# Late value products of key chunks 0 and 1 as three one-pass products of high and low halves, in an attention and mixture-of-experts kernel on one core

## The chip, the cores and the metric

One core of a Trainium2 chip. The metric is the device time of one execution in microseconds (us). Engines are named as the profile names them: PE is TensorE (PEld its weight loads), DVE VectorE, ACT ScalarE, POOL GpSimd, SP the queue that issues DMAs.

## The reference

32 heads (4 batches of 8) of 576 positions and 64 dimensions go through attention with a mask of 64-wide blocks; the result goes through a gated MLP with a one-step token shift, and then through a mixture of 8 experts of which each token uses one.

```python
    scores = scale * np.matmul(q, k.transpose(0, 1, 3, 2))
    mask = block_i >= block_j            # blocks of 64 positions
    scores = np.where(mask, scores, -1000000000.0)
    attn = np.exp(scores - np.max(scores, axis=-1, keepdims=True))
    attn = attn / (np.sum(attn, axis=-1, keepdims=True) + 1e-09)
    x = np.matmul(attn, v)               # then 512 wide per token
...
    k = np.maximum(xk @ w_k, 0.0)        # xk, xr: x mixed with the token before
    x = (1.0 / (1.0 + np.exp(-(xr @ w_r)))) * (k * k @ w_v)
...
    h = np.maximum(x[b, s] @ w1[e], 0.0)
    out[b, s] = p[e] * (h @ w2[e])
```

## The kernel before, in words

The program has three stages one behind the other: attention (32 heads, the first 200 us or so), the MLP, the experts. Each engine has its own hand-written order of instructions, and semaphores alone tie them together; nothing is scheduled by a planner. The change is in the attention stage.

A head `i` has five key chunks: four of 128 keys and one of 64. Its queries are 576 columns. Scores are made transposed (keys on partitions, queries along the row), so that chunk `c` needs only queries from `128 c` on. In PE's order, head `i` runs:

- `head_scores(i, ...)` (L708, L709): per piece one product of the rounded halves `hi` and one of `aug` (the low half of q, the row maximum and the mask), both in the one-pass type fp32r. The five pieces are chunk 0 for queries 0 to 255, chunk 0 from 256 on, chunk 1 (448 columns), chunk 2 (320 columns), and chunks 3 and 4 (192 and 64 columns).
- between them `head_row(i + 1)` (L694), which turns the row maxima of head i+1 into a row, and `head_max(i + 2, ...)` (L683, L686): rough scores of head i+2 in four groups, from which DVE takes the row maxima. Group 3 (L686, two products of 288 columns) goes into banks that groups 0 and 1 used, so it waits until DVE has reduced group 1.
- `head_pv(i, ...)` (L730): the product of the values with the exponentials, in full fp32. `PV` lists its seven products as (chunk, from query, to query); the early ones (queries under 256) and the late ones (from 256 on) go to two PSUM banks.

ACT in head `i`: `copy_out(i-1, 1)` (L1080) takes the late bank of the head before to `o_raw`; `head_exp(i)` (L1059) makes `pT`, the exponentials, in five pieces; `cast_tops(i+3)` (L1095) rounds q and k of head i+3 into `aug`; `split_wm_hi` (L1089) rounds a piece of an MLP weight (heads 4 to 30); `copy_out(i, 0)` takes the early bank. DVE: `copy_row(i+1)` (L1284), reductions (L1273, L1276) of the rough scores of head i+2 out of PSUM, `split_wm_lo` (L1308, heads 5 on), `cast_hi(i+3)` (L1295) and `split_q_lo(i+3)` (L1300), which read SBUF, a reciprocal of the sums (L1289). POOL: `split_k(i+3)` (L517), low half of k, after DVE's L1300 of that head; then `normalise(i-3)` (L526), which multiplies the output of head i-3 with its inverse sums into `xT`. SP issues the loads; the inverse sums go through DRAM (`spread_sums`, `store_inv`, `load_inv`).

`head_pv` waits for `row_copied` of head i+1, and `head_row(i+1)` for the maxima of that head, so a late DVE holds PE at those places and at group 3 of `head_max`.

Of the kernel before, what the change touches and what calls it, by code (L numbers as in the profile page):

```python
# [5 lines left out]
F32 = mybir.dt.float32  # L6
# [3 lines left out]
R32 = mybir.dt.float32r  # L10
ALU = mybir.AluOpType
ACT = mybir.ActivationFunctionType
AX = mybir.AxisListType
P = 128


def attention_moe_program(nc, qkT, v, mu_k, mu_r, w_k, w_v, w_r, w_gate9, w1, w2, out):

    NHEAD, _, _, S = qkT.shape
    DH = qkT.shape[1] // 2  # L20
# [7 lines left out]
    CH = (S + P - 1) // P  # L28
# [25 lines left out]
    with ExitStack() as ctx:  # L54
# [53 lines left out]
        mark = top["work"]  # L108
# [3 lines left out]
        P_AT = [sum(S - P * j for j in range(c)) for c in range(CH + 1)]  # L112
# [6 lines left out]
        v_sb = place("work", "v_sb", [P, 2, CH, 4 * DH])  # L119
# [5 lines left out]
        sums = place("work", "sums", [BLK, 2, S // BLK])  # L125
        inv = place("work", "inv", [P, S])
        pT = place("work", "pT", [P, 2, P_AT[CH]])
        attention_end, top["work"] = top["work"], mark

        xm = [[None, None], [None, None]]  # L130
        xm[0][1] = place("work", "xm_k_lo", [P, DC, NT], R32)
# [13 lines left out]
        assert max(top["work"], attention_end) <= top["w_mlp"] - 4 * DC * NT  # L145
        top["work"] = top["w_mlp"] - 4 * DC * NT
        xm[0][0] = place("work", "xm_k_hi", [P, DC, NT], R32)
        top["work"] = mark

        top["x"] = x_mark  # L150
# [124 lines left out]
        def third_at(j):  # L275
# [3 lines left out]
        ps = psum("ps", [P, 8, 512])  # L279


        names = ("pool_set const_done aug_made aug_copied aug_masked aug_set tops_cast hi_cast q_split k_split max_scores max_reduced max_row row_copied "
                 "scores_t exp_done pv_done o_copied sums_chain norm_done wm_is_hi wm_split xm_tmp xm_summed xm_is_hi "
                 "xm_split k_done relu_done ksq_done ksq_is_hi ksq_split r_done rexp_done sig_done v_done y_done "
                 "rows_done lg_sums logits_read ytok_done chain pre_dve pre_pe first_known slot_0 slot_1 ranks_read rt_dve rt_pe rt_exp shifted p_known p_stored slots_known exps_known turns_known tables o_half "
                 "weights_ready we_is_hi we_split xgt_ps xgt_is_hi xgt_done h_done relu_h ht_ps ht_is_hi ht_done "
                 "o_done o_scaled idx_copied waits_alone mu_loaded xm0_is_hi xm0_split").split()
        (pool_set, const_done, aug_made, aug_copied, aug_masked, aug_set, tops_cast, hi_cast, q_split, k_split, max_scores, max_reduced, max_row, row_copied,
         scores_t, exp_done, pv_done, o_copied, sums_chain, norm_done, wm_is_hi, wm_split, xm_tmp, xm_summed,
         xm_is_hi, xm_split, k_done, relu_done, ksq_done, ksq_is_hi, ksq_split, r_done, rexp_done, sig_done, v_done, y_done,  # L290
         rows_done, lg_sums, logits_read, ytok_done, chain, pre_dve, pre_pe, first_known, slot_0, slot_1, ranks_read, rt_dve, rt_pe, rt_exp, shifted, p_known, p_stored, slots_known, exps_known, turns_known,
         tables, o_half, weights_ready, we_is_hi, we_split, xgt_ps, xgt_is_hi, xgt_done, h_done, relu_h, ht_ps, ht_is_hi,
# [3 lines left out]
        def two(name):  # L296
            return [sem(f"{name}{k}") for k in range(2)]

        qk_loaded, v_loaded, row_loaded, sums_spread, inv_stored, inv_loaded = [
            two(n) for n in ("qk_loaded", "v_loaded", "row_loaded", "sums_spread", "inv_stored", "inv_loaded")]  # L300
# [49 lines left out]
        MAXB, OUTB = 3, 6  # L350
# [150 lines left out]
        def _(pool):  # L501
# [2 lines left out]
            nc.gpsimd.affine_select(out=ident[:, :], in_=ident[:, :], pattern=[[-1, P]], compare_op=ALU.not_equal,  # L504
                                    fill=1.0, base=0, channel_multiplier=1).then_inc(const_done, 1)
            nc.gpsimd.memset(xT[:, :, 0:1], 0.0)
            nc.gpsimd.memset(v_sb[:, :, :, :].rearrange("p j c (a d) -> p (j c) a d", d=DH)[:, :, 0:4:3, :], 1.0).then_inc(pool_set, 1)

            def alone():
# [3 lines left out]
            def split_k(i):  # L513

                pool.wait_ge(q_split, i + 1)
                alone()
                nc.gpsimd.tensor_tensor(hi[i % NBUF][DH:P, KEY, :], qk_raw[DH:P, i % 2, 1, :],  # L517
                                        hi[i % NBUF][DH:P, KEY, :].bitcast(F32), ALU.subtract).then_inc(k_split, 1)
                pool.wait_ge(k_split, i + 1)

            def normalise(i):

# [12 lines left out]
            pool.wait_ge(pool_set, 3)  # L535

            for i in range(NHEAD):
                if i + NBUF < NHEAD:
                    split_k(i + NBUF)
                if i >= NBUF:  # L540
                    normalise(i - NBUF)
# [27 lines left out]
            for bb in range(B):  # L569
                at, grp = bb * S % G, bb * S // G  # L570
# [95 lines left out]
        def _(pe):  # L666
            mm = nc.tensor.matmul
# [47 lines left out]
            def head_pv(i, pieces):  # L715
# [4 lines left out]
                for k in pieces:  # L720
# [11 lines left out]
                    if k in (2, 6):  # L732
                        last.then_inc(pv_done, 1)

            pe.wait_ge(const_done, 2)
            pe.wait_ge(aug_set, 1)
            head_max(0, (0, 1, 2, 3))
            head_row(0)
            pe.wait_ge(aug_copied, 16 * (NBUF - 1))
            head_max(1, (0, 1, 2, 3))  # L740
            for i in range(NHEAD):
                ahead = i + 2 < NHEAD
                head_scores(i, (0, 1))
                if i + 1 < NHEAD:
                    head_row(i + 1)
                if ahead:
                    head_max(i + 2, (0,))
                head_scores(i, (2, 3, 4))
                if ahead:
                    head_max(i + 2, (1,))  # L750
                head_pv(i, (0, 1))
                if ahead:
                    head_max(i + 2, (2,))
                head_pv(i, (2, 3))
                if ahead:
                    head_max(i + 2, (3,))
                head_pv(i, (4, 5, 6))
# [299 lines left out]
        def _(act):  # L1057
# [6 lines left out]
            def head_exp(i):  # L1064

                wait(act, pv_done, 2 * (i - 1))
                for j, piece in enumerate(PIECES):
                    act.wait_ge(scores_t, 5 * i + j + 1)
                    for c, q0, q1, col in piece:
                        rows, at = min(P, S - c * P), P_AT[c] - c * P  # L1070
                        last = exp(pT[0:rows, i % 2, at + q0:at + q1], ps[0:rows, PBANK[j], col:col + q1 - q0], scale=SCALE)
                    last.then_inc(exp_done, 1)

            def copy_out(i, half):

# [186 lines left out]
        def _(dve):  # L1262
# [101 lines left out]
            def xm_lo(s, w):  # L1364
# [2 lines left out]
                vec.tensor_tensor(xm[w][1][:, :, :], xsum[w][:, :, :], xm[w][0][:, :, :].bitcast(F32),  # L1367
                                  ALU.subtract).then_inc(xm_split, 1)

            for i in range(NHEAD):  # L1370
                if i + 1 < NHEAD:
                    copy_row(i + 1)
                if i + 2 < NHEAD:
                    head_reduce(i + 2, 0)
                if WFIRST < i:
                    split_wm_lo(i - 1 - WFIRST)
                if i + NBUF < NHEAD:
                    cast_hi(i + NBUF)
# [402 lines left out]
```

## Time and profile before

| | |
|---|---|
| median of 3 runs | 785.57 us (783.55 to 785.67) |
| the profiled execution | 783.86 us |
| its span, first to last instruction | 782.1 us |
| mean granted TensorE clock | 0.992 |
| PE, PEld busy | 96%, 84% of the span |
| DVE, ACT, POOL busy | 61%, 45%, 23% of the span |

A line of the profile names the source line, engine, operation, output tile and input tiles. A matmul in fp32 is recorded as two matmuls with their own weight loads; one in fp32r as one. The starts of matmuls are measured and their ends are modelled, so the distance from one start to the next tells what a matmul costs.

### The profile page before, as it was taken

The page shows a single profiled execution, that of the slowest core. Times are in us where ns is not written, and L with a number is a line of the kernel's source. Part 1 is how long each engine was busy: PE and PEld are TensorE (multiplying, and loading weights), DVE is VectorE, ACT ScalarE, POOL GpSimd, SP SyncE. Part 2 cuts the span into 40 slices and gives each one's busy share as a digit, 9 for nine tenths or more (in the row PEclk, how much of TensorE's full clock was granted, in tenths as well). Part 3 has the DMA queues.
Part 4 walks back from the last instruction along what each step waited for, and adds up shares of the span by engine and source line. Part 5 has one row for each costly group of instructions (what it writes and reads, how often), then busy time and mean ns, then how long its engine had stood idle before and what let it go on. Part 6 is the DMA issues. An engine that isn't in the chain of part 4 may idle for free.

```text
span 782.1 us, 13312 instructions
## 1 busy us (share of the span) xinstructions
PE 752.9 (96%) x4026; PEld 656.9 (84%) x4027; DVE 476.4 (61%) x848; ACT 350.3 (45%) x673; POOL 182.5 (23%) x211
## 2 busy tenths in 40 slices
PE   5999999999999999999999999989999999999993
PEld 4788788777889999999999998778888788888882
DVE  8777777878487775848478696622223745453261
ACT  4677677766662625335161333122123644353350
POOL 3244554454200000000020000123223232323221
PEclk9999999999999999999999999999999999999997
DMA  5666756552000010010101071167110176431000
GB/s 163 202 188 183 226 191 183 176 155 72 24 9 1 1 41 1 1 40 1 41 1 41 1 263 47 41 232 280 41 32 27 40 254 231 148 135 39 27 13 9
DMA packets 43061, 74.39 MB, mean 95 GB/s; under 512 B 10061, under 2 KB 20470, under 8 KB 43012
## 3 DMA queue, kind: packets, MB, share of 16 engines
q1 hardware_dynamic: 38676, 64.30, 24.5%
q0 software_dynamic: 4336, 9.47, 3.5%
q8 instruction: 27, 0.44, 0.2%
q14 instruction: 22, 0.18, 0.1%
HBM read 65.31 MB, written 10.57 MB: 97 GB/s over the span
## 4 chain that ended last, share of the span: by engine, by line
PE 93%; DVE 3%; ACT 1%; issue 1%; ACTq 0%; POOL 0%; DVEq 0%; POOLq 0%
PE ps L777 21%; PE ps L778 21%; PE ps L779 21%; PE ps L730 12%; PE ps L708 4%; PE ps L709 3%; PE ps L683 3%; PE ps L923 2%; PE ps L767 2%; PE ps L686 2%; PE ps L844 1%; ACT we_hi L1201 1%; PE ps L694 0%; DVE negm L1273 0%; DVE ksq L1354 0%
## 5 line engine op out<-in xcount | busy, mean ns | idle before, releaser
L730 PE MATMUL ps<-pT,v_sb 128*128 128x320 f32 (+4 forms) x448 | 112.4, 374 | 0.0
L730 PEld LDWEIGHTS ps<-pT,v_sb 128*128 128x128 f32 (+1 forms) x448 | 76.6, 193 | 19.1 <-issue 8.0
L777 PE MATMUL ps<-we_hi,hT_hi 128*128 (+1 forms) x176 | 73.3, 417 | 2.0 <-DVE o_sb L1727 1.3
L777 PE MATMUL ps<-we_hi,xgT_hi 128*128 (+1 forms) x176 | 70.4, 400 | 1.4 <-issue 1.4
L778 PE MATMUL ps<-we_lo,xgT_hi 128*128 (+1 forms) x176 | 69.7, 396 | 0.0
L779 PE MATMUL ps<-we_hi,xgT_lo 128*128 (+1 forms) x176 | 69.6, 395 | 0.0
L778 PE MATMUL ps<-we_lo,hT_hi 128*128 (+1 forms) x176 | 69.4, 394 | 0.0
L779 PE MATMUL ps<-we_hi,hT_lo 128*128 (+1 forms) x176 | 69.3, 394 | 0.0
L1222 ACT ACTIVATE hT_hi<-ps 128x512 fp32r<-128x512 f32 x44 | 26.1, 598 | 94.4 <-PE ps L923 50.5
L517 POOL TENSOR_TENSOR hi<-qk_raw,hi 64x576 fp32r<-64x576 f32 x32 | 44.8, 1401 | 96.7 <-DVE aug L1300 96.5
L777 PE MATMUL ps<-xm_k_hi,wk_hi 128*128 128x384 f32 x192 | 65.2, 340 | 1.6 <-DVE ksq L1414 1.6
L777 PE MATMUL ps<-ksq_hi,wv_hi 128*128 128x384 f32 x192 | 66.0, 344 | 0.7 <-DVE yT L1449 0.7
L1059 ACT ACTIVATE pT<-ps 128x256 f32<-128x256 f32 (+2 forms) x192 | 61.0, 391 | 9.6 <-PE ps L709 9.3
L778 PE MATMUL ps<-ksq_lo,wv_hi 128*128 128x384 f32 x192 | 64.9, 338 | 0.0
L779 PE MATMUL ps<-ksq_hi,wv_lo 128*128 128x384 f32 x192 | 64.9, 338 | 0.0
L779 PE MATMUL ps<-xm_k_hi,wk_lo 128*128 128x384 f32 x192 | 64.6, 336 | 0.0
L778 PE MATMUL ps<-xm_k_lo,wk_hi 128*128 128x384 f32 x192 | 64.4, 335 | 0.0
L1620 DVE TENSOR_TENSOR we_lo<-we_raw,we_hi (+1 forms) x48 | 55.6, 1219 | 10.9 <-ACT we_hi L1201 10.9
L1435 DVE RECIPROCAL sig<-sig 128x384 f32<-128x384 f32 x24 | 61.3, 2553 | 0.8
L1159 ACT ACTIVATE relu_k<-ps 128x384 f32<-128x384 f32 x48 | 23.6, 491 | 81.0 <-PE ps L779 81.0
L708 PE MATMUL ps<-hi 128*128 128x256 f32 (+2 forms) x192 | 56.4, 311 | 1.9 <-ACT pT L1059 1.9
L1633 DVE TENSOR_TENSOR hT_lo<-ps,hT_hi 128x512 fp32r<-128x512 f32 x44 | 30.0, 685 | 44.2 <-ACT hT_hi L1222 44.2
(254 smaller groups left out, 1676.1 us busy)
## 6 DMA issues: line engine op xcount, KB each, us to landing
we_raw<-w SPq DMA_DIRECT2D x12, 2048.0 KB, 11.7
qk_raw<-qkT SPq DMA_DIRECT2D x32, 576.0 KB, 3.8
v_sb<-v SPq DMA_DIRECT2D x16, 320.0 KB, 5.1
inv<-inv_scratch SPq DMA_DIRECT2D x32, 144.0 KB, 4.4
y_scratch<-ytok SPq DMA_DIRECT2D x6, 768.0 KB, 3.4
wk_raw<-w_k SPq DMA_DIRECT2D x8, 256.0 KB, 5.3
wv_raw<-w_v SPq DMA_DIRECT2D x8, 256.0 KB, 4.9
wr_raw<-w_r SPq DMA_DIRECT2D x4, 256.0 KB, 4.9
```

The source lines that it names most:

```text
L517: nc.gpsimd.tensor_tensor(hi[i % NBUF][DH:P, KEY, :], qk_raw[DH:P, i % 2, 1, :], hi[i % NBUF][DH:P, KEY, :].bitcast(F32), ALU.subtract).th ...
L708: mm(dst, hi[b][:, KEY, keys], hi[b][:, Q, q0:q1], start=True, stop=False)
L730: last = mm(ps[:, OUTB + half, q0 - 256 * half:q1 - 256 * half], v_sb[0:rows, j % 2, c, cols], pT[0:rows, i % 2, at + q0:at + q1], start=( ...
L777: mm(dst, a_hi, b_hi, start=(k == 0), stop=False)
L778: mm(dst, a_hi, b_lo, start=False, stop=False)
L779: return mm(dst, a_lo, b_hi, start=False, stop=(k == n - 1))
L1059: return nc.scalar.activation(dst, src, ACT.Exp, **kw)
L1159: nc.scalar.activation(relu_k[:, f % 2, :], ps[:, KB + f % 2, 0:NT], ACT.Relu).then_inc(relu_done, 1)
L1222: nc.scalar.activation(hT_hi[:, half * FC // 2:(half + 1) * FC // 2, :].rearrange("p f t -> p (f t)"), ps[:, 3 + half, :], ACT.Copy).then_ ...
L1435: vec.reciprocal(sig[:, d, :], sig[:, d, :]).then_inc(sig_done, 1)
L1620: vec.tensor_tensor(we_lo[part][:, third], we_raw[part][:, third], we_hi[part][:, bass.ds(slot_at(j) + k * EPIECE, EPIECE)].bitcast(F32), ...
L1633: vec.tensor_tensor(hT_lo[:, fs, :].rearrange("p f t -> p (f t)"), ps[:, 3 + half, :], hT_hi[:, fs, :].rearrange("p f t -> p (f t)").bitca ...
```

## The change

For heads 0 to 27 (`NSPLIT`) the two late products of chunks 0 and 1 (320 queries each) are no longer one fp32 product each. The exponentials and the values are written as a high half (rounded to fp32r) and a low half (the rest), and each product becomes three fp32r products: high by high, low by high, high by low. The low by low part is left out. ACT makes the high half of the exponentials (`p_hi`), POOL the low half in place (`pT_lo` lies on `pT`), DVE both halves of the values once per pair of heads. The late bank is now begun by chunk 2, and the six new products come last in the head, behind group 3 of `head_max`. Line numbers of the changed kernel are larger: L709 and L712 there are L683 and L686 here, L734 and L735 are L708 and L709, L775 and L782 are L730.

```diff
+            def split_p(i):
+                for c in range(2):
+                    pool.wait_ge(p_is_hi, 2 * i + c + 1)
+                    alone()
+                    nc.gpsimd.tensor_tensor(late_half(pT_lo, i)[:, c, :], late_half(pT, i)[:, c, :], p_hi[:, c, :].bitcast(F32),
+                                            ALU.subtract).then_inc(p_split, 1)
+                    pool.wait_ge(p_split, 2 * i + c + 1)
...
             for i in range(NHEAD):
+                if i < NSPLIT:
+                    split_p(i)
                 if i + NBUF < NHEAD:
                     split_k(i + NBUF)
...
+            def head_pv_late(i):
+                cols, end = slice((1 - i % 2) * P, (1 - i % 2) * P + P), ps[:, OUTB + 1, 0:LATE]
+                pe.wait_ge(v_split, i // 2 + 1)
+                for c in range(2):
+                    pe.wait_ge(p_split, 2 * i + c + 1)
+                    mm(end, v_hi[:, c, cols], p_hi[:, c, :], start=False, stop=False)
+                    mm(end, v_hi[:, c, cols], late_half(pT_lo, i)[:, c, :], start=False, stop=False)
+                    last = mm(end, v_lo[:, c, cols], p_hi[:, c, :], start=False, stop=(c == 1))
+                last.then_inc(pv_done, 1)
...
+                if i < NSPLIT:
+                    head_pv_split(i, (0, 1))
+                    head_max(i + 2, (2,))
+                    head_pv_split(i, (2, 3, 4))
+                    head_max(i + 2, (3,))
+                    head_pv_late(i)
+                    continue
                 head_pv(i, (0, 1))
...
                     last.then_inc(exp_done, 1)
+                    if i < NSPLIT and j in (2, 3):
+                        act.wait_ge(exp_done, 5 * i + j)
+                        nc.scalar.activation(p_hi[:, j - 2, :], late_half(pT, i)[:, j - 2, :], ACT.Copy).then_inc(p_is_hi, 1)
...
+            def split_v(j):
+                wait(dve, pv_done, 4 * j)
+                dve.wait_ge(v_loaded[j % 2], 16 * (j // 2) + 16)
+                mine = slice(DH, 3 * DH)
+                vec.tensor_copy(v_hi[:, :, mine], v_sb[:, j % 2, 0:2, mine]).then_inc(v_is_hi, 1)
+                dve.wait_ge(v_is_hi, j + 1)
+                vec.tensor_tensor(v_lo[:, :, mine], v_sb[:, j % 2, 0:2, mine], v_hi[:, :, mine].bitcast(F32),
+                                  ALU.subtract).then_inc(v_split, 1)
             for i in range(NHEAD):
+                if i % 2 == 0 and i < NSPLIT:
+                    split_v(i // 2)
                 if i + 1 < NHEAD:
                     copy_row(i + 1)
```

The other new lines are `head_pv_split`, the same fp32 products without the two late ones (chunk 0 now in one piece for queries under 256), new buffers, four more memsets of POOL at the start (the columns of ones and zeros of `v_hi` and `v_lo`), and PE's wait for them.

The order of instructions shows the new places. PE, from the early value products to the scores of the next head, before:

```order
L730 MATMUL ps<-pT,v_sb 128x256
L730 MATMUL ps<-pT,v_sb 128x320
L683 MATMUL ps<-aug_71 128x512
L730 MATMUL ps<-pT,v_sb 128x128
L730 MATMUL ps<-pT,v_sb 128x320
L686 MATMUL ps<-aug_71 64x288 x2
L730 MATMUL ps<-pT,v_sb 128x320
L730 MATMUL ps<-pT,v_sb 128x192
L730 MATMUL ps<-pT,v_sb 128x64
L708 MATMUL ps<-hi_68 128x256
```

and of the change, from group 2 of the rough scores on:

```order
L709 MATMUL ps<-aug_71 128x512
L782 MATMUL ps<-pT,v_sb 128x320
L782 MATMUL ps<-pT,v_sb 128x192
L782 MATMUL ps<-pT,v_sb 128x64
L712 MATMUL ps<-aug_71 64x288 x2
L791 MATMUL ps<-p_hi,v_hi 128x320
L792 MATMUL ps<-pT_lo,v_hi 128x320
L793 MATMUL ps<-p_hi,v_lo 128x320
L791 MATMUL ps<-p_hi,v_hi 128x320
L792 MATMUL ps<-pT_lo,v_hi 128x320
L793 MATMUL ps<-p_hi,v_lo 128x320
L734 MATMUL ps<-hi_68 128x256
```

Two fp32 products of 320 columns are gone, six one-pass ones stand at the end, and group 3 of the rough scores has all the fp32 products before it. POOL in the steady state of the heads, before:

```order
L517 TENSOR_TENSOR hi_72<-qk_raw,hi_72 64x576
L526 TENSOR_TENSOR xT<-o_raw,inv 64x576
L517 TENSOR_TENSOR hi_68<-qk_raw,hi_68 64x576
L526 TENSOR_TENSOR xT<-o_raw,inv 64x576
L517 TENSOR_TENSOR hi_70<-qk_raw,hi_70 64x576
```

and of the change:

```order
L541 TENSOR_TENSOR pT_lo<-pT,p_hi 128x320 x2
L532 TENSOR_TENSOR hi_72<-qk_raw,hi_72 64x576
L550 TENSOR_TENSOR xT<-o_raw,inv 64x576
L541 TENSOR_TENSOR pT_lo<-pT,p_hi 128x320 x2
L532 TENSOR_TENSOR hi_68<-qk_raw,hi_68 64x576
```

Each head has two more subtractions on POOL, ahead of the two it had. DVE in an even head of the change, from its first new row:

```order
L1447 CAST v_hi<-v_sb 128x2x128
L1449 TENSOR_TENSOR v_lo<-v_sb,v_hi 128x2x128
L1356 CAST m_rows<-ps 5x128
L1345 TENSOR_REDUCE negm<-ps 128x1 x2
L1380 TENSOR_TENSOR wk_lo<-wk_raw,wk_hi 128x374
L1367 CAST hi_70<-qk_raw 128x1152
L1372 TENSOR_TENSOR aug_71<-qk_raw,hi_70 64x576
L1345 TENSOR_REDUCE negm<-ps 128x1 x2
```

The first two rows are new, ahead of the copy of the row of maxima; the rest is as before.

## Rows read from the trace of the kernel before

**Rows 1.** The chain that ended last, by engine; the stretch of heads by windows.

```profile
PE 93%; DVE 3%; ACT 1%; issue 1%; ACTq 0%; POOL 0%; DVEq 0%; POOLq 0%
12.00:170.00 158.00, 157.74 (x868) 125.83 (x869) 120.74 (x260) 110.06 (x259) 71.58 (x52) 1.00 0.59 186
```

**Rows 2.** Timeline of PE in one head: start us, us, engine, line.

```profile
151.22 0.39 PE L708 MATMUL ps<-hi 128*128 128x256 f32 x1
...
152.21 0.37 PE L708 MATMUL ps<-hi 128*128 128x448 f32 x1
152.42 0.37 PE L709 MATMUL ps<-aug 69*128 69x448 f32 x1
...
153.47 1.13 PE L730 MATMUL ps<-pT,v_sb 128*128 128x256 f32 x4
154.20 0.63 PE L683 MATMUL ps<-aug 69*128 69x512 f32 x1
154.67 0.93 PE L730 MATMUL ps<-pT,v_sb 128*128 128x128 f32 x4
155.48 0.48 PE L686 MATMUL ps<-aug 69*64 69x288 f32 x2
...
157.12 0.39 PE L708 MATMUL ps<-hi 128*128 128x256 f32 x1
```

**Rows 3.** Timeline of DVE in the same head.

```profile
152.13 0.28 DVE L1284 CAST m_rows<-ps 5x128 fp32r<-5x128 f32 x1 [1.27 <-PE ps L694]
...
152.95 0.54 DVE L1308 TENSOR_TENSOR wv_lo<-wv_raw,wv_hi 128x374 fp32r<-128x374 f32 x1
153.42 0.76 DVE L1295 CAST hi<-qk_raw 128x1152 fp32r<-128x1152 f32 x1
154.21 0.75 DVE L1300 TENSOR_TENSOR aug<-qk_raw,hi 64x576 fp32r<-64x576 f32 x1
154.89 1.14 DVE L1273 TENSOR_REDUCE negm<-ps 128x1 fp32r<-128x384 f32 x2
...
156.07 0.69 DVE L1276 TENSOR_REDUCE negm<-ps 64x1 fp32r<-64x576 f32 x1
```

**Rows 4.** Timeline of POOL in the same head.

```profile
155.13 1.40 POOL L517 TENSOR_TENSOR hi<-qk_raw,hi 64x576 fp32r<-64x576 f32 x1 [2.88 <-DVE aug L1300]
156.74 1.41 POOL L526 TENSOR_TENSOR xT<-o_raw,inv 64x576 f32<-64x576 f32 x1 [0.20 <-POOL hi L517]
```

**Rows 5.** Timeline of ACT in the same head.

```profile
151.33 0.53 ACT L1080 ACTIVATE o_raw<-ps,eps 128x320 f32<-128x320 f32 x1 [1.41 <-PE ps L730]
...
152.82 1.19 ACT L1059 ACTIVATE pT<-ps 128x448 f32<-128x448 f32 x4 [0.28 <-PE ps L709]
...
154.95 0.51 ACT L1089 ACTIVATE wv_hi<-wv_raw 128x374 fp32r<-128x374 f32 x1
155.35 0.47 ACT L1080 ACTIVATE o_raw<-ps,eps 128x256 f32<-128x256 f32 x1
```

**Rows 6.** POOL by line and shape: a narrow operation.

```profile
L534 POOL TENSOR_SCALAR omu<-mu 128x8 f32<-128x8 f32 x1 | 0.5, 506 | 1.0 <-DMA idw<-w_gate 1.0
```

**Rows 7.** Timelines of POOL and DVE where the two meet, first meeting.

```profile
187.85 1.43 POOL L526 TENSOR_TENSOR xT<-o_raw,inv 64x576 f32<-64x576 f32 x1 [0.20 <-POOL xT L526]
188.34 1.34 DVE L1308 TENSOR_TENSOR wv_lo<-wv_raw,wv_hi 128x374 fp32r<-128x374 f32 x1
```

**Rows 8.** The same, second meeting.

```profile
204.88 1.09 DVE L1361 TENSOR_TENSOR xm_k_lo<-ksq,xm_k_hi 128x384 fp32r<-128x384 f32 x2
205.48 1.76 POOL L526 TENSOR_TENSOR xT<-o_raw,inv 64x576 f32<-64x576 f32 x1 [4.34 <-DMA inv<-inv_scratch]
```

**Rows 9.** PE after a long wait, and the windows (PE, PEld, DVE, ACT, POOL, PEclk, DMA share, GB/s) behind it.

```profile
195.65 0.41 PE L708 MATMUL ps<-hi 128*128 128x320 f32 x1 [1.86 <-ACT pT L1059]
197.00:199.00 2.00, 2.00 (x7) 1.51 (x6) 1.53 (x4) 0.49 (x2) 0.00 (x0) 0.50 0.23 76
199.00:201.00 2.00, 2.00 (x9) 1.34 (x8) 0.00 (x0) 1.48 (x3) 1.25 (x1) 0.83 0.00 0
```

More of the change, by code:

```diff
@@ L127, in attention_moe_program, with late_half @@
         pT = place("work", "pT", [P, 2, P_AT[CH]])
-        attention_end, top["work"] = top["work"], mark
+        NSPLIT = NHEAD - 4
+        LATE = S - 256
+        pT_lo = nc.alloc_sbuf_tensor_at("pT_lo", [P, 2, P_AT[CH]], R32, offset=top["work"] - 4 * 2 * P_AT[CH])
+        attention_end = top["work"]
+        p_hi = place("work", "p_hi", [P, 2, LATE], R32)
+        v_hi = place("work", "v_hi", [P, 2, 4 * DH], R32)
+        v_lo = place("work", "v_lo", [P, 2, 4 * DH], R32)
+        split_end, top["work"] = top["work"], mark
+        def late_half(tile, i):
+            return tile[:, i % 2, 256:256 + 2 * (S - P)].rearrange("p (c q) -> p c q", c=2)[:, :, 0:LATE]
         xm = [[None, None], [None, None]]
@@ L147, in attention_moe_program @@
         xm[0][0] = place("work", "xm_k_hi", [P, DC, NT], R32)
+        assert split_end <= top["work"]
         top["work"] = mark
@@ L282, in attention_moe_program @@
         names = ("pool_set const_done aug_made aug_copied aug_masked aug_set tops_cast hi_cast q_split k_split max_scores max_reduced max_row row_copied "
-                 "scores_t exp_done pv_done o_copied sums_chain norm_done wm_is_hi wm_split xm_tmp xm_summed xm_is_hi "
+                 "scores_t exp_done p_is_hi p_split v_split v_is_hi pv_done o_copied sums_chain norm_done wm_is_hi wm_split xm_tmp xm_summed xm_is_hi "
                  "xm_split k_done relu_done ksq_done ksq_is_hi ksq_split r_done rexp_done sig_done v_done y_done "
@@ L288, in attention_moe_program @@
         (pool_set, const_done, aug_made, aug_copied, aug_masked, aug_set, tops_cast, hi_cast, q_split, k_split, max_scores, max_reduced, max_row, row_copied,
-         scores_t, exp_done, pv_done, o_copied, sums_chain, norm_done, wm_is_hi, wm_split, xm_tmp, xm_summed,
+         scores_t, exp_done, p_is_hi, p_split, v_split, v_is_hi, pv_done, o_copied, sums_chain, norm_done, wm_is_hi, wm_split, xm_tmp, xm_summed,
          xm_is_hi, xm_split, k_done, relu_done, ksq_done, ksq_is_hi, ksq_split, r_done, rexp_done, sig_done, v_done, y_done,
@@ L506, in _ @@
             nc.gpsimd.memset(xT[:, :, 0:1], 0.0)
+            for half in (0, 3):
+                nc.gpsimd.memset(v_hi[:, :, half * DH:half * DH + DH].bitcast(F32), 1.0)
+                nc.gpsimd.memset(v_lo[:, :, half * DH:half * DH + DH].bitcast(F32), 0.0)
             nc.gpsimd.memset(v_sb[:, :, :, :].rearrange("p j c (a d) -> p (j c) a d", d=DH)[:, :, 0:4:3, :], 1.0).then_inc(pool_set, 1)
@@ L733, in head_pv, with head_pv_split @@
                         last.then_inc(pv_done, 1)
+            def head_pv_split(i, pieces):
+                j, cols = i // 2, slice((1 - i % 2) * P, (1 - i % 2) * P + P)
+                early, end = ps[:, OUTB, :], ps[:, OUTB + 1, 0:LATE]
+                for c in pieces:
+                    if c == 0:
+                        pe.wait_ge(v_loaded[j % 2], 16 * (j // 2) + 16)
+                        pe.wait_ge(row_copied, min(i + 2, NHEAD))
+                        wait(pe, o_copied, 2 * i - 1)
+                    if c == 2:
+                        wait(pe, o_copied, 2 * i)
+                    at = P_AT[c] - c * P
+                    if c < 2:
+                        pe.wait_ge(exp_done, 5 * i + (1, 3)[c])
+                        last = mm(early[:, c * P:256], v_sb[:, j % 2, c, cols], pT[:, i % 2, at + c * P:at + 256],
+                                  start=(c == 0), stop=(c == 1))
+                        if c == 1:
+                            last.then_inc(pv_done, 1)
+                    else:
+                        rows, q0 = min(P, S - c * P), max(256, c * P)
+                        pe.wait_ge(exp_done, 5 * i + (4, 5, 5)[c - 2])
+                        mm(end[:, q0 - 256:], v_sb[0:rows, j % 2, c, cols], pT[0:rows, i % 2, at + q0:at + S],
+                           start=(c == 2), stop=False)
+            def head_pv_late(i):
[6 more added lines that the diff above has]
+                    last = mm(end, v_lo[:, c, cols], p_hi[:, c, :], start=False, stop=(c == 1))
+                last.then_inc(pv_done, 1)
             pe.wait_ge(const_done, 2)
             pe.wait_ge(aug_set, 1)
+            pe.wait_ge(pool_set, 2)
             head_max(0, (0, 1, 2, 3))
```

## The prediction

> **What bounds the kernel now.** I read the chain of waits first: 93% of it is PE, and in the stretch of heads PE is busy 157.74 of 158.00 us, DVE 120.74, ACT 110.06 and POOL 71.58 [rows 1]. So TensorE sets the attention stage, and an edit that shortens PE pays only while the others keep up. Next the timeline of PE: one head lasts from 151.22 to 157.12, that is 5.90 us [rows 2]. In the others' timelines of that head, DVE waits 1.27 us for the row product, ACT 1.41 and 0.28 us, POOL 2.88 us for L1300 [rows 3 to 5]. By time alone there is room for new work. The last view is where operations of DVE and POOL meet, because busy shares don't show what two engines do to each other [rows 7, 8].
>
> **PE's own gain.** Below I count from the head's start, 151.22. From 153.47 to 154.67 stand fp32 products of 256 and 320 columns and one of 512 in one pass; the one-pass rate is 0.21 us for 448 columns (152.21 to 152.42), 0.47 ns per column, so that 0.24 of the 1.20 us is the 512, and 0.96/576 = 1.67 ns per column is the fp32 rate. From 154.67 to 155.48 it is 0.81/448 = 1.81 [rows 2]. The two late products therefore cost 1.07 to 1.16 us, and six one-pass ones of 320 columns 6 x 0.15 = 0.90. The gain is 0.17 to 0.26 us per head; I take 0.22, which would be 28 x 0.22 = 6.2 us if nothing else moved. The weight loads stay behind products of this width; the order of the other products moves them, and I cost that at nothing (cover: the products of 288 and 320 columns in front of the new ones).
>
> **ACT.** Two copies of 320 columns: L1089, 374 columns, takes a slot of 0.40 us (154.95 to 155.35), so 0.35 each, 0.70 per head against 1.69 us of waits [rows 5]. The exponentials of chunks 3 and 4 come 0.7 us later, near 3.5, and their products stand at 3.6 or later: hidden. If that cover were gone, it would cost a few tenths of a us in every head.
>
> **POOL.** A subtraction of 576 columns takes 1.40 us [rows 4]. In proportion 320 columns are 0.78. A narrow operation of 8 columns takes 0.51 us [rows 6]; if that much were fixed, 320 columns would cost 0.51 + 0.89 x 320/576 = 1.00. I take 0.80, nearer to the rows of the same operation. POOL then works 2 x 0.80 + 1.40 + 1.41 = 4.4 us per head, by itself under 5.7. DVE gets in each even head a cast of 256 columns (0.76/1152 ns per column and some start: 0.25) and a subtraction of 256 (0.54 for 374 columns: 0.40). The four memsets and PE's new wait at the start lie in time in which POOL waits anyway: nothing. SP's queue keeps its transfers and order; its waits on POOL's split and on the inverse sums have the time of a head in hand.
>
> **What the two do to each other.** This is the step that decides. At 188.34 a subtraction of DVE with both inputs in SBUF takes 1.34 us in place of 0.54, while a multiplication of POOL runs to 189.28 [rows 7, 3]: it got going 0.14 us before POOL's recorded end (189.68 - 0.54 = 189.14). The other way round, POOL's operation at 205.48 takes 1.76 in place of 1.41, beside a DVE pair that ends at 205.97 [rows 8, 4]. They don't share; one stands until the other is done, all but some 0.13 us. In the steady head of before this never shows: POOL's two operations (3.91 to 5.31, 5.52 to 6.93) lie beside reductions from PSUM, and L1308, L1295 and L1300 are done at 3.74 [rows 3, 4]. The new POOL operations come at 2.5, when ACT has the high halves, right in the middle of L1295 and L1300.
>
> No row shows a cast (L1295, L1447) meet POOL, so its price lies between nothing and the whole. It goes through a column in 0.66 ns (0.76/1152), the subtraction next to it in 1.30 (0.75/576) [rows 3]: twice the rate, which suggests that it too uses the second way to SBUF. I take the whole. The Trainium skill, page SBUF — State Buffer, section Who interferes with whom, says that VectorE and GpSimd share one port pair as an exclusive lock, held by VectorE operations with two SBUF inputs and by fp32 copies and casts in the two-port mode; by that rule the cast counts in full, as I count it, and a reader who keeps only to the rows has the rival on the casts below.
>
> The sum of what excludes each other, per pair of heads: DVE 2 x (0.54 + 0.76 + 0.75) + 0.25 + 0.40 = 4.75; POOL 2 x (1.40 + 1.41 + 1.60) = 8.82; together 13.6, or 6.8 us per head. (Before: 2.05 + 2.81 = 4.86 of 5.90, so it fitted.) With some 0.13 us saved at each of about ten handovers the floor is 6.15. So **the shared access becomes the bound** in place of PE.
>
> By the chain, in an odd head: row copy at 0.9 and L1308 on time; the cast 2.2 to 2.9, first split 2.8 to 3.6, L1300 3.5 to 4.2, second split 4.1 to 4.9, reduction of group 1 done at 4.7, group 3 of the rough scores at 4.7 (before: 4.26), then 0.32 + 0.90: 5.95. In an even head: DVE begins with the two v operations and copies the row at 1.05 to 1.33; the normalisation left over from the head before holds the port from 1.0 to 2.3, L1308 follows to 2.8, first split 2.7 to 3.5, cast to 4.1, second split to 4.8, L1300 to 5.4, group 1 reduced at 5.87, group 3 at 5.9, end at 7.1. The mean is 6.5. Between the chain (6.5) and the plain sum (6.8) I take 6.65 for heads 5 to 27: 23 x 0.75 = 17.3. Heads 0 to 4 have no L1308; without its 0.54 the chain gives about 5.95: 5 x 0.05 = 0.3. Heads 28 to 31 are as before. Sum: +17.6 on the profiled execution, 783.86 + 17.6 = 801.5. That execution lies 1.7 us under the median of the runs, 785.57; against the median it is 803. A measurement of this kernel can tell about 0.3%, 2.4 us, from no change.
>
> **The rivals.**
> - *The forecast, the port as the bound (0.62).* Its own range: 6.15 per head (+6) to 6.8 with splits of 1.00 us (6.8 + 0.4 = 7.2, 23 x 1.3 = +30 us): 791 to 816.
> - *The casts don't hold the port, or the engines fall into an order that hides it (0.15).* Then per pair 2 x 1.29 + 0.40 + 8.82 = 11.8, 5.9 per head with nothing saved, 5.3 with the handovers; PE's path of 5.68 decides again below that. In full: -6.2, 779.4, faster; half way: no change. It decides from the point where the reduction of group 1 is done before 4.4. For it: no row shows the cast meet POOL, and DVE and POOL both have waits now. Against: even without the casts the two subtractions of DVE meet two of POOL's in a place that had none. Faster 0.10, the same 0.05.
> - *The clock falls too (0.18).* PE waited 1.86 us before 195.65, and soon after the granted clock was 0.50 (1.2 in place of 2.4 GHz) for all of 197 to 199 and 0.83 on the mean of 199 to 201 [rows 9]: 2.0 + 2.0 x 0.17/0.50 = 2.7 us at half rate, and more ahead of 197. The even head of the chain makes PE wait 5.9 - 4.4 = 1.4 us. If each of 14 such waits brings 2.7 us or somewhat more at half rate, it loses 1.4 to 1.8 us of work, up to +25 on the forecast in all, less what PE had to wait anyhow: 815 to 828. For it: the row. Against: the wait is shorter, and PE is dense around it.
> - *Late exponentials or another chain (0.05):* a wait of 0.1 to 0.2 us per head on ACT or POOL eats the gain, with the port harmless: 785 to 790, slower by a little.
>
> That the change doesn't do what it says is no rival: the order shows six one-pass products in place of two fp32 ones in each of 28 heads.
>
> **How the numbers follow.** The likeliest case gives 803. The range 788 to 824 leaves out the faster case, the same, and the upper end of the clock case, together about 2 in 10. Faster 0.10, the same 0.05, slower 0.85.
>
> **What would show it.** In the profile of the changed kernel: spacing near 0.15 us for the new products; POOL's splits recorded longer than 0.8 us, or L1295 and L1300 (now L1367 and L1372) longer than 0.76 and 0.75 or late, on a mean of two heads; PE waiting in front of group 3 of the rough scores for a DVE reduction; even heads longer than odd ones by about 1 us; a granted clock of 1.00 from 20 to 200 us, else the clock rival. I am wrong if PE stays busy without gaps there and a head lasts 5.7 us, or if PE waits in front of the new products for POOL and not in front of group 3.

## The result, and the profile after

| | before | after |
|---|---|---|
| median of 4 runs | 785.53 us (783.55 to 785.67) | 809.68 us (807.05 to 815.42) |
| the profiled execution, its span | 783.86 us, 782.1 us | 807.05 us, 805.3 us |
| mean granted clock | 0.992 | 0.986 |
| ratio | | 1.0327, 95% interval 1.0305 to 1.0349 |

The change makes the kernel 3.3% slower. The last copy of a row of maxima, which DVE makes in head 30, starts at 194.3 us before and at 217.1 after; what follows takes 587.8 and 588.1 us. So 22.8 of the 23.1 us by which the span grows lie in the heads. The tile of that copy by name, of before and of after (count, shortest, median and longest in ns, first and last start in us):

```profile
L1284 DVE CAST m_rows<-ps x32: 271/279/280, 9.5 to 194.3; 5x128 fp32r<-5x128 f32 x32
```

```profile
L1356 DVE CAST m_rows<-ps x32: 271/278/281, 9.5 to 217.1; 5x128 fp32r<-5x128 f32 x32
```

The four executions of the changed kernel are spread wider than those of before, and the two longest, 812.14 and 815.42 us, have the lowest mean granted clocks, 0.981 and 0.978; they left no trace, so more is not known of them.

Below, **us per head** is the distance from the copy of the row of head 5 to that of head 27, over 22: (169.83 - 39.93)/22 = 5.905 before, (191.14 - 41.48)/22 = 6.80 after.

The chain of work that ended last, of after (93% PE and 3% DVE in [rows 1]):

```profile
PE 76%; DVE 19%; issue 2%; ACT 1%; ACTq 0%; POOL 0%; DVEq 0%; POOLq 0%
```

A fifth of the path is now DVE. PE in after, from the end of an odd head through an even one (135.42 to 142.79) and an odd one (to 148.72): start us, us, engine, line, and in brackets the wait in front (before: [rows 2]).

```profile
134.21 0.48 PE L712 MATMUL ps<-aug 69*64 69x288 f32 x2 [0.31 <-DVE negm L1345]
134.54 0.31 PE L791 MATMUL ps<-p_hi,v_hi 128*128 128x320 f32 x1
134.68 0.31 PE L792 MATMUL ps<-pT_lo,v_hi 128*128 128x320 f32 x1
...
135.42 0.28 PE L734 MATMUL ps<-hi 128*128 128x256 f32 x1
...
141.59 0.48 PE L712 MATMUL ps<-aug 69*64 69x288 f32 x2 [1.75 <-DVE negm L1345]
...
142.79 0.28 PE L734 MATMUL ps<-hi 128*128 128x256 f32 x1
...
148.72 0.28 PE L734 MATMUL ps<-hi 128*128 128x256 f32 x1
```

The new products are 0.15 us apart as costed. PE waits in front of group 3 of the rough scores, 0.31 us in the odd head and 1.75 in the even one, for DVE's reduction of group 1. DVE and POOL beside it, DVE first (before: [rows 3, 4]):

```profile
135.62 0.57 DVE L1447 CAST v_hi<-v_sb 128x256 fp32r<-128x256 f32 x1
136.22 0.43 DVE L1449 TENSOR_TENSOR v_lo<-v_sb,v_hi 128x256 fp32r<-128x256 f32 x1
136.57 0.27 DVE L1356 CAST m_rows<-ps 5x128 fp32r<-5x128 f32 x1
...
137.30 1.09 DVE L1380 TENSOR_TENSOR wr_lo<-wr_raw,wr_hi 128x410 fp32r<-128x410 f32 x1
138.31 1.42 DVE L1367 CAST hi<-qk_raw 128x1152 fp32r<-128x1152 f32 x1
139.77 1.30 DVE L1372 TENSOR_TENSOR aug<-qk_raw,hi 64x576 fp32r<-64x576 f32 x1
```

```profile
136.24 1.71 POOL L550 TENSOR_TENSOR xT<-o_raw,inv 64x576 f32<-64x576 f32 x1 [0.20 <-POOL hi L532]
138.15 0.97 POOL L541 TENSOR_TENSOR pT_lo<-pT,p_hi 128x320 fp32r<-128x320 f32 x1 [0.20 <-POOL xT L550]
139.32 1.13 POOL L541 TENSOR_TENSOR pT_lo<-pT,p_hi 128x320 fp32r<-128x320 f32 x1 [0.20 <-POOL pT_lo L541]
141.23 1.42 POOL L532 TENSOR_TENSOR hi<-qk_raw,hi 64x576 fp32r<-64x576 f32 x1 [0.78 <-DVE aug L1372]
```

These rows show one of the two engines at work at a time, in turns. The cast L1367, 0.76 us before, takes 1.42 and ends at 139.73; less its own 0.76 it got going at 138.97, 0.15 before the recorded end of POOL's split at 139.12. L1372 takes 1.30 in place of 0.75. POOL's normalisation takes 1.71 in place of 1.41, beside `v_lo`. The same by group, of after (behind the bar the busy us and the mean ns of one; the means of L1372 and L1367 were 751 and 757 before):

```profile
L541 POOL TENSOR_TENSOR pT_lo<-pT,p_hi 128x320 fp32r<-128x320 f32 x56 | 59.8, 1067 | 31.5 <-ACT p_hi L1144 23.1 <-POOL pT_lo L541 5.7 <-POOL xT L550 2.5
L1372 DVE TENSOR_TENSOR aug<-qk_raw,hi 64x576 fp32r<-64x576 f32 x32 | 38.9, 1215 | 1.1
L1367 DVE CAST hi<-qk_raw 128x1152 fp32r<-128x1152 f32 x32 | 31.8, 993 | 1.0 <-PE ps L735 0.8
```

### The profile page after: what moved, and what is told of

It is laid out like the page before. It is cut to its first block, busy times and chain, and to the rows that moved or that the text cites. A ratio compares the mean times of both kernels' runs of the same rounds, so it can differ in the third digit from the quotient of the medians.

```text
span 805.3 us, 13666 instructions
## 1 busy us (share of the span) xinstructions
PE 750.6 (93%) x4082; PEld 666.8 (83%) x4083; DVE 518.9 (64%) x876; ACT 368.0 (46%) x729; POOL 247.4 (31%) x271
## 4 chain that ended last, share of the span: by engine, by line
PE 76%; DVE 19%; issue 2%; ACT 1%; ACTq 0%; POOL 0%; DVEq 0%; POOLq 0%
PE ps L846 20%; PE ps L848 19%; PE ps L847 19%; DVE aug L1372 5%; DVE hi L1367 4%; DVE negm L1345 3%; PE ps L992 2%; PE ps L836 2%; PE ps L712 2%; PE ps L734 1%; PE ps L735 1%; PE ps L756 1%; DVE sig L1519 1%; PE ps L913 1%; PE ps L793 1%
## 5 line engine op out<-in xcount | busy, mean ns | idle before, releaser
L1128 ACT ACTIVATE pT<-ps 128x256 f32<-128x256 f32 (+2 forms) x192 | 66.6, 388 | 7.5 <-PE ps L735 6.8
L541 POOL TENSOR_TENSOR pT_lo<-pT,p_hi 128x320 fp32r<-128x320 f32 x56 | 59.8, 1067 | 31.5 <-ACT p_hi L1144 23.1
L636 POOL DMA_INDIRECT out<-o_sb,idx_out x22 | 22.5, 1025 | 145.1 <-DVE o_sb L1811 145.1
L550 POOL TENSOR_TENSOR xT<-o_raw,inv 64x576 f32<-64x576 f32 x32 | 49.5, 1547 | 28.0 <-DMA inv<-inv_scratch 22.5
```

Source lines behind the costliest of these rows:

```text
L541: nc.gpsimd.tensor_tensor(late_half(pT_lo, i)[:, c, :], late_half(pT, i)[:, c, :], p_hi[:, c, :].bitcast(F32), ALU.subtract).then_inc(p_sp ...
L550: nc.gpsimd.tensor_tensor(xT[own, i // 2, 1:1 + S], o_raw[own, i % NOUT, :], inv[own, :], ALU.mult).then_inc(norm_done, 1)
L1128: return nc.scalar.activation(dst, src, ACT.Exp, **kw)
```

## The experiments

Four kernels (the second to the fifth below) leave parts of the computation out, as their expectations say. That changes which expert a token goes to, and so the length of the last stage, up to 20 us. For those only the us per head count, and their medians stand in brackets.

| kernel | us per head | median, us | ratio to before, 95% |
|---|---|---|---|
| before | 5.905 | 785 | |
| the change | 6.80 | 809.68 | 1.0305 to 1.0349 |
| PE's order alone | 5.76 | 780.33 | 0.9907 to 0.9956 |
| no split on POOL | 5.89 | (806.0) | |
| values split once | 6.80 | (807.41) | |
| POOL fills, doesn't read | 6.00 | (807.61) | |
| PE's and ACT's work alone | 5.54 | (776.21, one run) | |
| other DVE order | 8.52 | 852.94 | 1.0829 to 1.0931 |
| splits on DVE | 6.54 | 801.39 | 1.0172 to 1.0248 |
| PE's and DVE's order | 5.76 | 781.66 | 0.9947 to 0.9979 |
| short product inside | 5.91 | 784.74 | 0.9981 to 1.0005 |
| PE's order, short product padded | 5.57 | 775.89 | 0.9861 to 0.9899 |
| short product padded alone | 5.57 | 775.72 | 0.9860 to 0.9898 |

The theory, called A in the expectations: DVE's operations on SBUF (L1308, L1295, L1300 by the numbers of before, and the two on the values) and POOL's exclude each other, and POOL's two subtractions make their sum the bound. Its rivals: the new order on PE costs the time; DVE's split of the values ahead of the row copy does; or POOL's sheer duration in the chain does.

**PE's order alone.** The late products stay fp32 and only change places; the splits on POOL and DVE and the two copies on ACT are taken out.

```diff
-                if i < NSPLIT:
-                    split_p(i)
...
-                pe.wait_ge(v_split, i // 2 + 1)
                 for c in range(2):
-                    pe.wait_ge(p_split, 2 * i + c + 1)
-                    mm(end, v_hi[:, c, cols], p_hi[:, c, :], start=False, stop=False)
-                    mm(end, v_hi[:, c, cols], late_half(pT_lo, i)[:, c, :], start=False, stop=False)
-                    last = mm(end, v_lo[:, c, cols], p_hi[:, c, :], start=False, stop=(c == 1))
+                    last = mm(end, v_sb[:, (i // 2) % 2, c, cols], late_half(pT, i)[:, c, :], start=False, stop=(c == 1))
...
-                if i % 2 == 0 and i < NSPLIT:
-                    split_v(i // 2)
```

> The change's order of PE alone: the two late products of chunks 0 and 1 stay fp32 and stand last in the head, nothing is split, ACT, DVE and POOL do what they did before. Theory A (one shared way to SBUF that DVE and POOL use one at a time is the bound of the changed heads): no operation of DVE or POOL is new, so 783 to 788 us, no change against before. Rival C (it is the new order of PE, with group 3 of the rough scores later, that costs): 800 us or more.

Measured: 780.33 us, 0.9931 of before, 5.76 us per head. The order doesn't cost, it gains 0.14 us per head. Neither the theory (783 to 788 us) nor the prediction, which had the order at nothing, foresaw that. The rival on the order falls.

**No split on POOL.**

```diff
-                if i < NSPLIT:
-                    split_p(i)
...
-                    pe.wait_ge(p_split, 2 * i + c + 1)
+                    pe.wait_ge(p_is_hi, 2 * i + c + 1)
...
-                    mm(end, v_hi[:, c, cols], late_half(pT_lo, i)[:, c, :], start=False, stop=False)
+                    mm(end, v_hi[:, c, cols], p_hi[:, c, :], start=False, stop=False)
```

> POOL's two subtractions per head are taken out; PE waits for ACT's high halves instead and multiplies them twice, so the low half of the exponentials is left out of the result and PE's work is the same. Theory A: L1372 back to 0.75 us and the cast to 0.76, no stall in front of group 3 of the rough scores, 5.7 us per head, 776 to 783 us, faster than before. Rival B (the split of the values on DVE, ahead of the row copy, is the main cost): still above 795 us.

Measured: 5.89 us per head, so with POOL's subtractions go 0.91 of the 6.80 us, as much as the whole loss of 0.90. That includes 0.20 for the falls of the clock (4.3 us in 22 heads, below), which are gone here too. Yet 5.7 was expected. By group, L1370 (L1372 of after) is back at 750 ns, and the cast of the values is not what it was costed at:

```profile
L1365 DVE CAST hi<-qk_raw 128x1152 fp32r<-128x1152 f32 x28 | 21.1, 752 | 2.0 <-PE ps L733 2.0
L1370 DVE TENSOR_TENSOR aug<-qk_raw,hi 64x576 fp32r<-64x576 f32 x28 | 21.0, 750 | 1.0
L1445 DVE CAST v_hi<-v_sb 128x256 fp32r<-128x256 f32 x13 | 15.0, 1153 | 1.4
```

The cast of the values stands beside POOL's normalisation and waits for it: 1.15 us in place of 0.28.

**Values split once.**

```diff
-                pe.wait_ge(v_split, i // 2 + 1)
+                pe.wait_ge(v_split, 1)
...
-                if i % 2 == 0 and i < NSPLIT:
-                    split_v(i // 2)
+                if i == 0:
+                    split_v(0)
```

> The values are split for the first pair of heads only (the other heads multiply by that pair's halves; their late sums are wrong). Theory A: 0.5 to 1.0 us less of the shared way per pair of heads, even heads become like odd ones (6.27 in place of 6.97 us): 14 x 0.7 = 10 us less, and with fewer stalls of PE perhaps the three falls of the clock go (4 us): 795 to 800 us. Rival B (the split of the values is the main cost): 785 us or less. If both engines only had too much work each, and no exclusion: no change, 807 to 812.

Measured: 6.80 us per head, no gain. The expectation missed. In its heads 5 to 27, 17 us lie at half clock against 10 in the change. At the price found below (4.3 us for the 10) the falls cost 7.2 us here, so that (7.2 - 4.3)/22 = 0.13 us per head, by this estimate, is what the missing split gives and the clock takes back. Beside POOL's subtractions the split of the values is worth little, and that it is the main cost falls. No gain is also what the third forecast said, by which nothing excludes anything; the next run decides on that one.

**POOL fills instead of subtracting.** The same place and a similar time, but POOL reads nothing from SBUF there. PE multiplies by the high half twice, as in the run without POOL's split.

```diff
-                    nc.gpsimd.tensor_tensor(late_half(pT_lo, i)[:, c, :], late_half(pT, i)[:, c, :], p_hi[:, c, :].bitcast(F32),
-                                            ALU.subtract).then_inc(p_split, 1)
+                    nc.gpsimd.memset(filler[:, :], 0.0)
+                    nc.gpsimd.memset(late_half(pT_lo, i)[:, c, :].bitcast(F32), 0.0).then_inc(p_split, 1)
```

> In place of each subtraction POOL fills two areas (256 and 320 columns) with zeros, some 0.7 us against 0.86, so that POOL is busy about as long at the same place but reads nothing from SBUF (the low half of the exponentials is left out, PE multiplies the high half twice). Theory A, if what DVE's subtractions wait for is POOL's reading: L1372 at 0.75 us, only the casts are ever held: 783 to 793 us. Theory A, if any POOL operation holds them all: 800 us or more. Rival D (no exclusion; POOL's duration in the chain to the late products is what costs): near 805 us, with PE waiting in front of the late products for POOL.

Measured: 6.00 us per head, 0.8 less than the change, with POOL's two fills at 0.50 and 0.39 us in the mean (0.31 and 0.37 where nothing holds them, against 0.86, the shortest subtraction of the change). By group:

```profile
L542 POOL MEMSET filler<- 128x256 f32 x54 | 27.2, 503 | 31.5 <-ACT p_hi L1145 26.2 <-POOL pT_lo L543 5.1 <-POOL xT L551 0.2
L543 POOL MEMSET pT_lo<- 128x320 f32 x55 | 21.6, 393 | 0.0
L1373 DVE TENSOR_TENSOR aug<-qk_raw,hi 64x576 fp32r<-64x576 f32 x28 | 21.0, 751 | 1.0
L1450 DVE TENSOR_TENSOR v_lo<-v_sb,v_hi 128x256 fp32r<-128x256 f32 x13 | 17.9, 1379 | 0.4
```

L1373 stands beside the fills and isn't touched; `v_lo` stands beside the normalisation, which reads, and is held (1.38 in place of 0.43). So what a subtraction of DVE waits for is POOL's reading, and POOL's time in the chain is worth 0.11 us per head at most (6.00 less the 5.89 without any split on POOL). The rivals by which nothing excludes anything fall. The Trainium skill, page SBUF — State Buffer, section Who interferes with whom, says that a VectorE instruction with two SBUF inputs contends with GpSimd instructions that read SBUF and not with those that only write; this run agrees, 0.751 us beside fills and 1.30 beside subtractions. The cast of q and k is another matter. In one head of the same run:

```profile
126.60 0.75 DVE L1368 CAST hi<-qk_raw 128x1152 fp32r<-128x1152 f32 x1
127.38 0.75 DVE L1373 TENSOR_TENSOR aug<-qk_raw,hi 64x576 fp32r<-64x576 f32 x1
126.66 1.00 POOL L543 MEMSET pT_lo<- 128x320 f32 x1
127.83 0.31 POOL L542 MEMSET filler<- 128x256 f32 x1 [0.18 <-POOL pT_lo L543]
```

The fill at 126.66, beside the cast, takes 1.00 us in place of 0.37; the one at 127.83, beside the subtraction, takes its own 0.31. So a cast and a fill exclude each other, and in this run it is mostly the fill that waits. POOL's normalisation and `split_k` still meet the values' split here, which is most of why it is 6.0 and not the 5.54 of the next run.

**PE's and ACT's work alone**: the edits of "no split on POOL" and "values split once" together.

> No split on POOL and the values split for the first pair only, with PE's and ACT's work as in the change (the low half of the exponentials and the right values of later pairs are left out, so the routing to experts and with it the last stage differ: only the attention stage is compared, by the mean distance of the row copies of heads 5 to 27, which was 5.905 us before, 6.80 after, 5.76 with the order alone and 5.89 without POOL's split). Theory A (the port): 5.50 to 5.60 us per head, PE without waits; what separates this from 5.89 is then the split of the values beside POOL's normalisation. Rival (ACT's two copies or the chain over them bound it): 5.7 or more.

Measured, in one execution: 5.543 us per head, every distance 5.54 or 5.55. That is the change's gain on PE: 0.36 per head, 0.14 by the order and 0.22 by the one-pass products. ACT's copies cost nothing. The split of the values alone takes 5.89 - 5.54 = 0.35 of it back. And the change's own 6.80 can be added up: 5.54, PE's waits in front of group 3 of (0.31 + 1.75)/2 = 1.03, and 0.20 for the clock make 6.77.

**Another order on DVE.**

```diff
-                if i % 2 == 0 and i < NSPLIT:
-                    split_v(i // 2)
...
+                if i + 2 < NHEAD:
+                    head_reduce(i + 2, 1)
                 if i + NBUF < NHEAD:
                     cast_hi(i + NBUF)
                     split_q_lo(i + NBUF)
+                if i % 2 == 0 and i < NSPLIT:
+                    split_v(i // 2)
                 if i + 2 < NHEAD:
-                    head_reduce(i + 2, 1)
                     head_reduce(i + 2, 2)
```

> The full change with another order on DVE: the reduction of group 1 ahead of the cast and subtraction of head i+3, the split of the values behind them. If only the chain over the late reduction cost the time: 5.6 to 5.8 us per head, 777 to 783 us. If the sum of what excludes each other is the bound (theory A): shorter waits of PE in front of group 3, but 6.2 to 6.5 us per head, 793 to 802 us.

Measured: 852.94 us, 8.52 per head, far outside both forecasts. The wait in front of group 3 is gone, and a longer one has come. Timelines of DVE, POOL and PE:

```profile
133.59 1.60 DVE L1449 TENSOR_TENSOR v_lo<-v_sb,v_hi 128x256 fp32r<-128x256 f32 x1
```

```profile
133.52 1.39 POOL L532 TENSOR_TENSOR hi<-qk_raw,hi 64x576 fp32r<-64x576 f32 x1 [0.78 <-DVE aug L1372]
```

```profile
135.25 0.41 PE L791 MATMUL ps<-p_hi,v_hi 128*128 128x320 f32 x1 [2.45 <-DVE v_lo L1449]
...
137.23 0.57 PE L734 MATMUL ps<-hi 128*128 128x448 f32 x1
```

L1372 releases POOL's `split_k`, which starts 0.07 us ahead of `v_lo`; the late products wait 2.45 us for it, and the product of 448 columns at 137.23 takes 0.37 us to the next in place of 0.21: the clock has gone to its lower level. In heads 5 to 27 it is there for 75 of 188 us. This is what the clock rival of the prediction describes, a fall in each pair of heads, though behind waits of 2.45 and not of 1.4 us. The three parts add up: PE's path of 5.54, half of 2.45 for the wait, and for the clock, by an estimate, at most half of 75 us over 22 heads, 1.7, make 8.5.

**Both subtractions of the exponentials on DVE**, behind the cast of head i+3; the reduction of group 1 and the split of the values stand ahead of that cast. `split_p` is now DVE's (`vec.tensor_tensor`), and POOL has none.

```diff
+                if i + 2 < NHEAD:
+                    head_reduce(i + 2, 1)
+                if i % 2 == 0 and i < NSPLIT:
+                    split_v(i // 2)
                 if i + NBUF < NHEAD:
                     cast_hi(i + NBUF)
+                if i < NSPLIT:
+                    split_p(i)
+                if i + NBUF < NHEAD:
                     split_q_lo(i + NBUF)
                 if i + 2 < NHEAD:
-                    head_reduce(i + 2, 1)
```

> As the kernel before this one in the list, and both subtractions of the exponentials on DVE in place of POOL, about 0.45 us each in place of 0.86. Exclusive sum per head: 2.05 + 0.9 + 0.4 on DVE, 2.81 on POOL, 6.1 less some 0.4 at handovers; DVE's own work 5.7. Theory A: 5.7 to 6.1 us per head, 779 to 791 us. If the work on DVE delays PE through the reductions: above 6.2.

Measured: 801.39 us, 6.54 per head, above the 5.7 to 6.1 of the theory; the other forecast, that the work on DVE delays PE, came. Timeline of DVE in an odd head:

```profile
139.84 1.12 DVE L1369 TENSOR_TENSOR wr_lo<-wr_raw,wr_hi 128x410 fp32r<-128x410 f32 x1
140.88 0.55 DVE L1334 TENSOR_REDUCE negm<-ps 128x1 fp32r<-128x384 f32 x1
141.34 0.74 DVE L1356 CAST hi<-qk_raw 128x1152 fp32r<-128x1152 f32 x1
142.01 0.88 DVE L1435 TENSOR_TENSOR pT_lo<-pT,p_hi 128x320 fp32r<-128x320 f32 x2
142.82 0.74 DVE L1361 TENSOR_TENSOR aug<-qk_raw,hi 64x576 fp32r<-64x576 f32 x1
...
145.20 0.28 DVE L1345 CAST m_rows<-ps 5x128 fp32r<-5x128 f32 x1 [0.32 <-PE ps L709]
```

DVE has no gap but 0.32 us, and PE waits for its last reduction in front of the row product, some 0.45 and 0.65 us in turns. The sum of what excludes each other fell, and DVE itself became the bound, helped by the half microsecond that its weight split (1.12 in place of 0.58) loses beside the normalisation.

**Order of PE and DVE, no splits** (PE's order alone with the DVE order above).

> No splits, the change's order on PE (5.76 us per head, ratio 0.993 alone) and the new order on DVE. PE had no waits in front of group 3 with the order alone, so the DVE order should change nothing: 779 to 782 us; 5.76 per head.

Measured: 5.76 per head and 781.66 us, as expected: the order on DVE changes nothing where PE has no wait to save.

**Where the order's 0.14 us come from.** The kernel before with the product of chunk 4, the short one, between those of chunks 2 and 3:

```diff
...
-                head_pv(i, (4, 5, 6))
+                head_pv(i, (4, 6, 5))
```

> The kernel before with one thing changed: the product of chunk 4 (64 keys, 64 queries) stands between those of chunks 2 and 3 and no longer last in the head. Question: where the 0.14 us per head of the order alone come from. Theory T (the short product has no cover for the weight load behind it, and the scores' first load of 128 columns is then bare): 5.78 to 5.85 us per head, 781 to 784 us. Rival (it is the merging of the two early value products): 5.90 per head, 784 to 786.

Measured: 5.91, no change. Its place among the late products isn't it. The rival named there, the merging of the two early products, had no run of its own. Then the shape of the short product: 128 keys in place of 64, with zeros. The edits for PE's order; the kernel before gets the same two, and PE's wait for the fill:

```diff
+            nc.gpsimd.memset(pT[:, :, P_AT[CH - 1]:P_AT[CH]], 0.0)
...
-                        rows, q0 = min(P, S - c * P), max(256, c * P)
+                        rows, q0 = P, max(256, c * P)
```

> The order alone, and the product of chunk 4 over 128 keys in place of 64, with zeros in the upper half of its exponentials (written once at the start, the values there are zeros too; the result is the same). In the trace of before, the weight load of the 64-row product stands 0.23 us bare each head. Theory T2 (it is bare because it has another number of rows than the load before it): 0.15 to 0.25 us per head less than the order alone, 5.52 to 5.61, 773 to 776 us. Rival (it is bare because the products around it are short): no change, 5.76 per head, 780 us.

> The kernel before with the padded product of chunk 4 alone. Theory T2: 5.65 to 5.75 us per head, 777 to 781 us. Rival as above: 5.90 per head, 784 to 786.

Measured: 775.89 us with the order, 775.72 without, 5.57 per head both, 1.2% faster than before. The first came as expected; the second gained more than the theory had (5.65 to 5.75 per head). One fill at the start takes 0.33 us per head away, and since the padded product is as short as before (64 columns), the number of its rows was what cost. Timelines of PE, first of the kernel before, then of the same with the padded product:

```profile
155.80 1.39 PE L730 MATMUL ps<-pT,v_sb 128*128 128x320 f32 x6
157.12 0.39 PE L708 MATMUL ps<-hi 128*128 128x256 f32 x1
157.34 0.28 PE L709 MATMUL ps<-aug 69*128 69x256 f32 x1
```

```profile
136.98 1.19 PE L731 MATMUL ps<-pT,v_sb 128*128 128x320 f32 x6
137.99 0.37 PE L709 MATMUL ps<-hi 128*128 128x256 f32 x1
```

The six records take 1.01 us in place of 1.32. The idle time in front of the weight loads of the value products in which PE waited for nothing that the profile shows ("issue"), by the tile of the values, was 8.0 us in 36 pieces before; here:

```profile
its engine sat idle before it (us, times) until:
  issue: 1.3, 7
```

The order's 0.14 us don't come on top. The starts in the traces show where they lie. In the kernel before, the first score product, right behind the short one, takes 0.22 us to the next (157.12 to 157.34), where it takes 0.12 in the change (135.42 to 135.54), and the fp32 record in front of group 3 takes 0.32 (the mean of 20 heads) where such a record otherwise takes 0.27. With the order alone four records of 320 columns stand in front of the scores, and nothing is lost:

```profile
155.79 1.24 PE L787 MATMUL ps<-pT,v_sb 128*128 128x320 f32 x4
156.63 0.53 PE L732 MATMUL ps<-hi 128*128 128x256 f32 x1
156.99 0.28 PE L733 MATMUL ps<-aug 69*128 69x256 f32 x1
```

1.20 us are four times 0.27 and 0.12. The short product, now in front of group 3, still takes its 0.36 us there but slows nothing behind it. So 0.10 us come from the product behind the short one and 0.05 from the one in front of group 3; why the group behind isn't slowed is open.

## Why the prediction was right or wrong

- *PE's own gain:* the one-pass products were costed at 0.22 us per head, and 5.76 - 5.54 gives 0.22. The step "the order of the other products moves them, and I cost that at nothing" was wrong by 0.14: PE's path is 5.54 and not 5.68. With the port as the bound it didn't reach the result.
- *The step that decides* held: DVE and POOL go one at a time, POOL's subtractions cost 0.91 us per head, the falls of the clock behind PE's longer waits (0.20) included, and the cast, whose price no row of before showed, waits in full (1.42 us). The rival that the casts don't hold the port falls with that row.
- *The chain* from one head's first score product to the next: 5.95 for an odd head and 7.1 for an even one. Measured are 148.72 - 142.79 = 5.93 and 142.79 - 135.42 = 7.37. The odd head came out as chained; the even one is 0.27 longer, since the cast of the values stood beside POOL's `split_k` (0.57 in place of 0.25), which put the row copy at 1.15 and not at 1.05, and POOL's two splits took 0.97 and 1.13 in place of 0.80. The mean, 6.65, is the number put in the sum. That was chosen between the chain's 6.5 and the plain 6.8 and not worked out, so that it fits this well is in part luck.
- *POOL's subtraction:* 0.86 us at the shortest, 0.80 in the sum.
- *The v operations:* cast 0.28 and subtraction 0.43 undisturbed, as costed (0.25, 0.40); 0.55 and 0.51 in the mean of the change.
- *Heads 0 to 4* cost 41.48 - 39.93 = 1.55 us, not 0.3, with the first `v_lo` at 1.62 us in place of 0.43, beside POOL's `split_k`: a meeting that the sum had left out for these heads.
- *The clock*, left out of the sum and kept as a rival (0.18): by the prediction's own sign, a granted clock of 1.00 from 20 to 200 us, it came true in part, with falls in three of the 11 even heads from 5 to 27. In those three the row copies are 8.41, 8.46 and 8.40 us apart and not 6.97: 1.45 each, 4.3 us. By windows of after (PE, PEld, DVE, ACT, POOL, PEclk, DMA share, GB/s):

```profile
124.00:127.00 3.00, 1.26 (x7) 0.84 (x6) 2.96 (x4) 1.85 (x4) 2.01 (x3) 0.96 0.95 303
127.00:130.00 3.00, 3.00 (x14) 2.85 (x13) 1.18 (x3) 0.85 (x2) 2.23 (x2) 0.50 0.38 126
```

- *The sum* said 801.5 us for the profiled execution, and it is 807.05. Of the 5.5 us the clock is 4.3, heads 0 to 4 are 1.2, and 0.8 lie behind head 27, where the sum had nothing. The term for heads 5 to 27 was too large by 0.8: 17.3 us, against (198.11 - 41.48) - (175.74 - 39.93) = 20.8 less the clock's 4.3, 16.5 (23 distances, from the copy of the row of head 5 to that of head 28). The median, forecast at 803, is 809.68; the two executions with a still lower clock are in it.

## What to carry to other kernels

Busy shares don't show what two engines do to each other. Before work is given to an idle POOL, add up those of DVE's and POOL's operations on SBUF that held each other here (subtractions and casts of DVE, subtractions and multiplications of POOL) over one period, and look in the trace for a place where they already meet. In this kernel 4.9 of 5.9 us per head were taken, and the change asked for 6.8. And take a gain apart by its edits: the order alone was faster, and a product with fewer rows than its neighbours had cost more (0.33 us per head) than the one-pass products could save (0.22).

## What the runs showed of the hardware that was not expected

- A value product over 64 rows among products over 128 costs 0.33 us per head more than one padded to 128 rows with zeros (5.905 to 5.573), though the padded one has twice the rows. The loss lies in front of its weight load, at its own two records and, in the kernel before, at the product behind it.
- An operation of DVE with two inputs in SBUF isn't held beside fills of POOL (0.751 us) and waits for a reading one nearly to its end (1.30 us); the wait stands inside the recorded duration. A cast of DVE and a fill do hold each other (a fill of 1.00 us in place of 0.37).
- The clock fell at waits of PE of 1.7 us in three of 11 even heads, though all 11 waits were alike (1.68 to 1.75 us), and in every pair of heads of the run with waits of 2.45 us. The three waits ended at 72.27, 126.77 and 181.35 us, every fourth even head. Why in those three is open.
